# Block 0 of the first layer moves to the second set of x buffers, and block 1 is split into its parts one phase earlier

## The reference

```python
def _attn_ref(x, weight):
    w = np.exp(weight - np.max(weight, axis=-1, keepdims=True))
    w = w / (np.sum(w, axis=-1, keepdims=True) + 1e-09)
    x_pad = np.concatenate([np.zeros((B, K - 1, D)), x], axis=1)
    idx = np.arange(S)[:, None] + np.arange(K)[None, :]
    x_unf = x_pad[:, idx, :].reshape(B, S, K, H, group)
    return np.einsum('hk,bskhg->bshg', w, x_unf).reshape(B, S, D)

def _moe_ref(x, w_in, w_out):          # first layer
    h = x @ w_in
    g = np.where(h >= 1, h, np.where(h <= -1, 0.0, (h + 1) ** 2 / 4))
    return g @ w_out

def _moe2_ref(x, w_in, w_out, s, b):   # second layer
    r = np.maximum(x @ w_in, 0.0)
    return (s * (r * r) + b) @ w_out
```

## Time and profile before

| what | value |
|---|---|
| median of 3 runs | 1155.81 us (1155.42 to 1156.33) |
| time of the profiled execution | 1150.71 us |
| span in the trace, first to last instruction | 1149.0 us |
| PE busy | 1125.8 us, 98% of the span |
| DVE busy | 947.9 us, 83% |
| ACT busy | 630.8 us, 55% |

### The profile page before, as it was taken

The page is one execution under the profiler, slowest core; times in us unless marked ns, Lnnn a source line. Parts: engine busy times, 40 slices in busy tenths (PEclk is TensorE's granted clock), DMA queues, the critical chain, the costliest instruction groups (busy, mean ns, idle before and its releaser), DMA issues.

```text
span 1149.0 us, 23218 instructions
## 1 busy us (share of the span) xinstructions
PE 1125.8 (98%) x9746; PEld 951.0 (83%) x9746; DVE 947.9 (83%) x858; ACT 630.8 (55%) x627; POOL 3.4 (0%) x16
## 2 busy tenths in 40 slices
PE   5999999999999999999999999999999999999998
PEld 3777878888888888888888888888888888888886
DVE  7998998978888798888888798887888878866665
ACT  4545655555565655555555555555555555565544
POOL 1000000000000000000000000000000000000000
PEclk8998999999999999999999999999999999999999
DMA  6002300100001000000000000000000000000000
GB/s 183 1 1 65 93 1 1 29 29 1 1 1 29 28 1 1 1 29 28 1 2 1 29 29 1 1 1 29 29 1 2 1 29 1 1 1 1 29 1 28
DMA packets 12423, 21.33 MB, mean 19 GB/s; under 512 B 1073, under 2 KB 5169, under 8 KB 12337
## 3 DMA queue, kind: packets, MB, share of 16 engines
q1 hardware_dynamic: 12256, 19.99, 6.1%
q0 software_dynamic: 64, 0.00, 0.0%
q10 hardware_dynamic: 16, 0.00, 0.0%
HBM read 13.70 MB, written 6.29 MB: 17 GB/s over the span
## 4 chain that ended last, share of the span: by engine, by line
PE 88%; DVE 8%; issue 3%; ACT 1%; DMA 0%; SPq 0%; DVEq 0%; ACTq 0%
PE acc L717 28%; PE h L670 23%; PE h L683 18%; PE acc_rem L732 18%; DVE g L445 3%; DVE g L453 1%; DVE mixed L502 1%; DMA xraw_rem<-in_x 0%; ACT g_hi L303 0%; DVE mixed_rem L516 0%; DVE mixed L516 0%; DVE up_lo L551 0%; DVE up_rem_lo L551 0%; DVE g_lo L463 0%; DVE dn_lo L551 0%
## 5 line engine op out<-in xcount | busy, mean ns | idle before, releaser
L303 ACT ACTIVATE g_hi<-g 128x1024 fp32r<-128x1024 f32 x128 | 135.8, 1061 | 218.8 <-DVE g L453 218.7
L447 DVE SCALAR_TENSOR_TENSOR g<-r,scale,h 128x1024 f32<-128x1024 f32 x128 | 161.9, 1278 | 69.5 <-ACT r L291 69.5
L305 ACT ACTIVATE g_hi<-g,shift 128x1024 fp32r<-128x1024 f32 x128 | 147.6, 1153 | 116.5 <-PE acc_rem L732 101.4
L717 PE MATMUL acc<-g_hi,dn_hi 64*128 64x512 f32 x1024 | 204.7, 389 | 0.4 <-issue 0.4
L732 PE MATMUL acc_rem<-g_lo,dn_rem 64*128 64x512 f32 x1024 | 204.6, 388 | 0.0
L732 PE MATMUL acc_rem<-g_hi,dn_rem 64*128 64x512 f32 x1024 | 204.6, 387 | 0.0
L717 PE MATMUL acc<-g_lo,dn_hi 64*128 64x512 f32 x1024 | 204.3, 388 | 0.0
L717 PE MATMUL acc<-g_hi,dn_lo 64*128 64x512 f32 x1024 | 204.0, 387 | 0.0
L466 DVE SCALAR_TENSOR_TENSOR g_lo<-g,shift,g_hi 128x1024 fp32r<-128x1024 f32 x128 | 164.1, 1282 | 43.6 <-ACT g_hi L305 43.4
L463 DVE TENSOR_TENSOR g_lo<-g,g_hi 128x1024 fp32r<-128x1024 f32 x128 | 156.8, 1225 | 42.9 <-ACT g_hi L303 42.7
L291 ACT ACTIVATE r<-h 128x1024 f32<-128x1024 f32 x128 | 128.1, 1026 | 109.6 <-PE h L683 97.5
(11 more groups left out here) (96 smaller groups left out, 1356.4 us busy)
## 6 DMA issues: line engine op xcount, KB each, us to landing
xraw<-in_x SPq DMA_DIRECT2D x7, 518.0 KB, 4.3
out<-res SPq DMA_DIRECT2D x7, 512.0 KB, 3.3
stage<-in_moe_w_out SPq DMA_DIRECT2D x6, 384.0 KB, 3.4
xraw_rem<-in_x SPq DMA_DIRECT2D x14, 129.5 KB, 4.0
out<-res_rem SPq DMA_DIRECT2D x7, 256.0 KB, 3.6
stage<-in_moe_w_in SPq DMA_DIRECT2D x2, 512.0 KB, 5.4
stage<-in_moe_w_in SPq DMA_DIRECT2D x4, 256.0 KB, 5.1
xraw<-in_x SPq DMA_DIRECT2D x1, 512.0 KB, 4.2
```

The source lines that it names most:

```text
L303: nc.scalar.activation(g_hi[k][:], g[k][:], ACT.Copy).then_inc(hi_ready, 1)
L305: nc.scalar.activation(g_hi[k][:], g[k][:], ACT.Identity, bias=shift[:, 0:1]).then_inc(hi_ready, 1)
L447: nc.vector.scalar_tensor_tensor(g[k][:], r[k][:], scale[:, 0:1], h[k][:], ALU.mult, ALU.mult).then_inc(h_used, 1)
L717: last = nc.tensor.matmul(acc[:, t, :], w[rows], v[rows, t, :], start=(j == 0 and side == 0 and n == 0), stop=(j == CH - 1 and side == 1 a ...
```

## The change

Phase 0 reads its block from X2 instead of X1. Since X1 is then free, ScalarE rounds the rem channels of block 1 at the end of j = 8 and the main channels at the end of j = 14, and VectorE makes the low part of the rem channels at the end of j = 9 (behind that chunk's tap) and that of the main channels at the end of j = 15. No instruction is added or removed, and all shapes stay.

```diff
@@ scalar
-            nc.scalar.activation(X1[0][:, 1, :], mixed_pe, ACT.Copy).then_inc(mixed_pe_hi, 1)
+            nc.scalar.activation(X2[0][:, 1, :], mixed_pe, ACT.Copy).then_inc(mixed_pe_hi, 1)
             act.wait_ge(mix_step, 2 * TAPS)
-            nc.scalar.activation(X1[0][:, 0, :], mixed[:, 0, :], ACT.Copy).then_inc(x_hi_done[0], 1)
-            round_mixed_rem(0, X1, None, interleaved=True)
+            nc.scalar.activation(X2[0][:, 0, :], mixed[:, 0, :], ACT.Copy).then_inc(x_hi_done[0], 1)
+            round_mixed_rem(0, X2, None, interleaved=True)
...
-            phase(0, None, 0, 0, 0, extras={n - 4: [lambda n=n: weights_hi(0, n)] for n in range(5, 8)},
-                  last=[lambda: round_mixed(1, X1, CH - 1), lambda: round_mixed_rem(1, X1, CH - 1)])
+            e = {n - 4: [lambda n=n: weights_hi(0, n)] for n in range(5, 8)}
+            e[8] = [lambda: round_mixed_rem(1, X1, None)]
+            e[14] = [lambda: round_mixed(1, X1, None)]
+            phase(0, None, 0, 0, 0, extras=e)
@@ vector
-            phase(0, None, 0, 0, extras=e, last=[lambda: low_mixed(1, X1), lambda: low_mixed_rem(1, X1)])
+            e[9].append(lambda: low_mixed_rem(1, X1))
+            e[15] = [lambda: low_mixed(1, X1)]
+            phase(0, None, 0, 0, extras=e)
@@ tensor
-            phase(0, None, 0, 0, X1, first_split, weights)
+            phase(0, None, 0, 0, X2, first_split, weights)
```

More of the change, by code:

```diff
@@ L608, in _ @@
             dve.wait_ge(mixed_pe_hi, 1)
-            nc.vector.tensor_tensor(X1[1][:, 1, :], mixed_pe, X1[0][:, 1, :].bitcast(F32),
+            nc.vector.tensor_tensor(X2[1][:, 1, :], mixed_pe, X2[0][:, 1, :].bitcast(F32),
                                     ALU.subtract).then_inc(mixed_pe_lo, 1)
             dve.wait_ge(x_hi_done[0], 1)
-            nc.vector.tensor_tensor(X1[1][:, 0, :], mixed[:, 0, :], X1[0][:, 0, :].bitcast(F32),
+            nc.vector.tensor_tensor(X2[1][:, 0, :], mixed[:, 0, :], X2[0][:, 0, :].bitcast(F32),
                                     ALU.subtract).then_inc(x_lo_done[0], 1)
             weights_lo(0, 1)
-            low_mixed_rem(0, X1)
+            low_mixed_rem(0, X2)
             for n in range(2, 5):
```

## The result

| | before | changed |
|---|---|---|
| median of 6 runs | 1155.66 us (1154.74 to 1156.33) | 1159.84 us (1159.31 to 1160.74) |
| ratio | | 1.0037, 95% interval 1.0024 to 1.0050 |
| profiled execution, span | 1150.71 us, 1149.0 us | 1160.25 us, 1158.5 us |

By the medians the change makes the kernel 4.2 us slower, and the interval (2.8 to 5.8 us) lies clear of zero; a median of 1160.3 was forecast.

A forecast was written before the change was run, and what follows sets the result against it. VectorE bounds phase 0, TensorE 160 to 1100 us; border delays are paid in full. The +4.5 us, already holding the rem pair's 1.43, takes 1155.81 to 1160.3 us; 8 in 10 range 1158.0 to 1162.6.

The forecast's parts named there:

- The other buffer set, 0: Phase 0 reading X2: removes a wait for `h_ready` that never ended last and changes no shape; gain 0.
- Rem pair on ScalarE hidden: ScalarE, j = 8: 1.27 us between relu 8 and relu 9, hidden behind VectorE with 1.0 us to spare.
- Rem pair on VectorE, +1.43: VectorE, j = 9: the pair lands where VectorE has no gap, moving all from j = 10 on by +1.43 us.
- Hold of relu 15: ScalarE, j = 14: relu 15 waits behind x_hi; `first` 15 at 97.07 instead of 93.42, VectorE hole 2.1 us.
- ScalarE doesn't hold relu 15: Rival at j = 14: relu 15 passes the waiting x_hi, 2.2 us sooner, +2.3 in all, 1158.1 us; chance 0.04.
- Place of x_lo: VectorE, j = 15: x_lo behind `first`, `low` and `second` at 100.52; TensorE's x_lo pass at 101.80.
- Clock: TensorE after the border's stand: half clock for 3.3 to 5.0 us, bound 6.84; middle of the two restarts +4.5 us.
- Paid in full: TensorE busy 939.48 of 940 us from 160 to 1100: any delay before that is paid in full.
- The sum: Whole kernel: +4.5 us, profiled execution 1155.2 us, median 1160.3 us; forecast's chance 0.75.
- the clock didn't fall in the timed runs before: Rival at the border: clock falls only after the change, adding 2.7 us: +7.2, 1163.0 us; chance 0.08.
- The 5.10 us between profiled and timed run: Median of the runs before lies 5.10 us above the profiled time; left as it is in the forecast.

The follow-up runs named there:

- the rem part alone: Against the kernel before, only the rem channels of block 1 split early, x_hi behind relu 15 and x_lo directly behind `first` 15: 1149.24 us, 0.9984.
- the filled pair: Changed kernel without and with x_hi put back behind relu 15, with 15 and 19 extra TensorE passes in the stand before x_lo: 1153.85 and 1155.16 us.
- x_lo first: Changed kernel, but VectorE makes x_lo directly behind `first` 15 instead of behind `low` 14 and `second` 15: 1152.93 us, 1.0018 of the kernel before.
- no hold: Changed kernel, but ScalarE rounds x_hi behind relu 15 again: 1155.54 us, 1.0041 of the kernel before; run again, 1155.92 us, 1.0034.
- the last group: Changed kernel and "no hold", each without and with extra TensorE passes, beside the kernel before (1152.07 us): 1156.66, 1155.92 without; 1155.16, 1153.85 us with.
- changed, filled kernel: Changed kernel plus 19 extra TensorE passes in the stand before x_lo: 1157.96 us, 1.0028 of the kernel before; run again, 1155.16 us, 1.0026.
- one tap earlier: Changed kernel with the main taps at j = 7 to 13 and x_lo at the end of j = 14: 1153.38 us, 0.9985 of the kernel before.

## Why the prediction was right

- *The other buffer set, 0*: shown (ratio 1.0001).
- *Rem pair on ScalarE hidden*: 1.27 us between relu 8 and relu 9, and `first` 9 (66.14, behind a tap) had no idle time. Right.
- *Rem pair on VectorE, +1.43*: 1.43 us in the trace, and the last tap 94.52 - 92.22 - 0.77 = 1.53 us later. Right. But the rem part alone, which I had at +0.4 us when I took the change apart, measured -1.8: it removes a stand, and in its trace the half clock was gone with it. In the whole change that gain doesn't appear, since both traces of it have half clock again around the stand of 4.84 us.
- *Hold of relu 15*: hole of 2.13 us where 2.1 was worked out. Shown by trace, and its effect by the filled pair (1.17 us at the first drain, 1.2 in the expectation). Here one step of the prediction was wrong, though the forecast didn't use it: the rival "ScalarE doesn't hold relu 15" was priced at 2.2 us less, which leaves out that `low` 14 then waits for its g_hi (0.94 us in the trace). The runs show 1.2. The Trainium skill (TensorE: Matmul & The Clock Gate, section "Architectural detail: the array is 16× 32×32, not 1× 128×128") says that ScalarE's and VectorE's queues are strictly first in, first out. The trace agrees: relu 15 starts at 96.79, behind x_hi at 95.83, and x_lo, whose x_hi was done at 96.89, stays behind three steps until 101.33.
- *Place of x_lo*: the x_lo pass at 102.60, or 101.83 without the 0.77; 101.80 was forecast. Putting x_lo first again took the cost to +2.1 us (+2.2 expected).
- *Clock*: the restart was followed by 4.5 us of half clock, between the 3.3 and 5.0 taken as bounds. That the middle fitted so well is in part luck: in the two traces of "no hold" half clock lasted 2.9 and 5.5 us behind the restart, past both bounds. relu 16 came 107.72 - 102.44 - 0.77 = 4.5 us later, the drain 4.4.
- *Paid in full*: at the second drain the changed kernel is 185.00 - 179.82 - 0.77 = 4.4 us late, as at the first. Right.
- *The sum*: +4.5 forecast, +4.2 measured by the medians, +4.6 by those of the last group. The forecast for the profiled execution, 1155.2, was 5.1 us too low (1160.25): 0.77 us were lost before the moved instructions, and 4.3 us are the slower pace behind the first drain.
- *The rival "the clock didn't fall in the timed runs before"* seems true in part, by the mean clocks: in some of the runs it hadn't. Against those runs the change looks dearer, and an edit that keeps the clock full gains less. That would help to explain why the gains in the timed runs (1.8, 1.0, 1.7) are below the 2.0 to 3.1 us seen at the first drain in the traces; 0.1 to 0.6 us more is given back in phase 1.
- *The 5.10 us between profiled and timed run*, which I left unexplained, fits in the main the pace of the steady part: from one drain to the next the changed kernel's trace has 69.43 us on average and the trace of the kernel before 69.11, which over the 13 steps behind the second drain makes 4.2 us. That the median came out right rests on this: the timed runs before and those of the change seem to have had the same, slower pace, which the prediction took for granted. No timed run of the kernel before in that group has a trace, and the cause of the pace stays open.

## What to carry to other kernels

A split moved ahead in an in-order queue is worth what its input allows: here ScalarE's rounding was put where it waited for the last tap with the activation of the next chunk behind it, and freeing the buffer bought nothing because no one had waited for it. Make the input early first (the main taps one chunk sooner, with x_lo behind them, turned +4.2 into -1.7 us), then move the consumer, and never put a side job with an unfinished input ahead of the work that feeds the bounding engine. Count TensorE's stands together with the clock that follows them: in the traces the kernel with stands of 1.60, 0.44 and 0.64 us had half clock, the one without the 0.64 had not, and was 2.0 us ahead at the first drain.

## What the runs showed of the hardware

The granted clock at the border was half (0.50) for 6.84 us in the kernel before and in the changed one, for 3.4 us in "x_lo first" and in one execution of "no hold", for 6.8 us in another, and not at all with stands of 1.60 and 0.44 us. It fell even in the middle of a stand (100.24 us in the changed kernel, which stood until 102.60), where it costs nothing.

The same stand did not always do the same. Early in phase 0 TensorE stands for 1.77 us in the kernel before and in the changed one:

```profile
27.57 0.50 PE L670 MATMUL h<-x_hi,up_hi 64*128 64x512 f32 x2 [1.77 <-DVE g L445]
```

```profile
28.33 0.62 PE L674 MATMUL h<-x_hi,up_hi 64*128 64x512 f32 x2 [1.77 <-DVE g L447]
```

The clock stayed at 1.00 in the first, and in the second it was 0.64 and 0.51 from 28 to 30 and 30 to 32 us. Of the traces of all kernels here with a stand of 1.76 or 1.77 us at this place, six kept the full clock and five had half clock for 3.4 us, though the order of the instructions up to here is the same in all eleven. So one trace with the clock full is no proof that an order keeps it full; the medians have to say it too.

Beside that, TensorE has more than one pace at a granted clock of 1.00. The changed, filled kernel took 1152.64 and 1152.85 us in two runs and 1157.74 to 1159.16 in seven; "one tap earlier" took 1147.40 once and 1152.25 to 1153.76 in twelve. Two profiles of one kernel, "no hold", from its first and its second group:

```profile
160.00:1100.00 940.00, 939.48 (x8266) 799.54 (x8264) 777.10 (x684) 522.88 (x505) 0.00 (x0) 1.00 0.04 11
```

```profile
160.00:1100.00 940.00, 939.48 (x8222) 806.42 (x8222) 774.05 (x681) 520.86 (x504) 0.00 (x0) 1.00 0.04 11
```

The three other traces of the last group lie between, with 8252 to 8254. The two ends are 5 us of this kernel apart, more than the change itself, so that one profiled execution against another would have told 9.5 us. What sets the pace no row tells.
